# The first 60 microseconds of an attention and two-MLP kernel: tau waited for later, other pieces, another closing of the norms

## The reference, cut to what matters

```python
# q, k, v: [1, 6016, 256] fp32, tau a scalar
qn = q / (norm(q, axis=1) + 1e-6)          # one norm per channel, over the 6016 tokens
kn = k / (norm(k, axis=1) + 1e-6)
s  = kn.T @ qn / tau                        # 256 x 256 scores
a  = softmax(s, rows)
x  = v @ a                                  # [6016, 256]
g  = x @ w_gate; x = (silu(g) * (x @ w_val)) @ w_out       # 256 -> 1536 -> 256
h  = x @ w_in;   out = (h * clip(h + 3, 0, 6) / 6) @ w_out2 # 256 -> 2048 -> 256
```

## Time and profile before

| what | us |
|---|---|
| median of three runs | 1160.79 |
| the profiled execution's own time | 1160.25 |
| its span | 1158.5 |
| TensorE busy in the span | 1150.3 |
| DVE, ScalarE, GpSimd busy | 709.6, 270.6, 76.6 |

### The profile page before, as it was taken

The page is one execution under the profiler, slowest core; times in us unless marked ns, Lnnn a source line. Parts: engine busy times, 40 slices in busy tenths (PEclk is TensorE's granted clock), DMA queues, the critical chain, the costliest instruction groups (busy, mean ns, idle before and its releaser), DMA issues.

```text
span 1158.5 us, 14651 instructions
## 1 busy us (share of the span) xinstructions
PE 1150.3 (99%) x5222; PEld 965.3 (83%) x5222; DVE 709.6 (61%) x1167; ACT 270.6 (23%) x450; POOL 76.6 (7%) x48
## 2 busy tenths in 40 slices
PE   8999999999999999999999999999999999999999
PEld 7888888888888888888888888888888888888998
DVE  5776764664665574485485476466557447548557
ACT  6731211211221221221121121122122122112122
POOL 5794000000000000000000000000000000000000
PEclk9999999999999999999999999999999999999999
DMA  9742020010002002002002002000100200100100
GB/s 347 243 127 55 1 37 0 0 31 5 0 3 33 0 0 36 0 0 36 0 0 36 0 0 34 3 0 9 28 0 0 36 0 0 32 0 0 19 1 14
DMA packets 106048, 33.77 MB, mean 29 GB/s; under 512 B 95664, under 2 KB 100400, under 8 KB 106032
## 3 DMA queue, kind: packets, MB, share of 16 engines
q1 hardware_dynamic: 105024, 32.51, 11.2%
q10 hardware_dynamic: 1008, 1.05, 0.3%
HBM read 27.39 MB, written 6.16 MB: 29 GB/s over the span
## 4 chain that ended last, share of the span: by engine, by line
PE 96%; ACT 1%; DMA 1%; DVE 1%; issue 0%; SPq 0%; ACTq 0%
PE psum L751 33%; PE psum L774 32%; PE psum L762 22%; PE psum L786 5%; PE psum L734 1%; ACT psum L387 1%; PE psum L804 1%; DMA tau_sb<-in_tau 1%; PE psum L654 1%; DVE sq_sum L482 1%; PE psum L802 0%; DMA qk_first<-in_q 0%; PE psum L818 0%; ACT parts_early L383 0%; ACT parts_late L383 0%
## 5 line engine op out<-in xcount | busy, mean ns | idle before, releaser
L774 PE MATMUL psum<-prod,down_w 128*128 128x512 f32 (+1 forms) x1644 | 410.2, 387 | 0.0
L774 PEld LDWEIGHTS psum<-prod,down_w 128*128 128x128 f32 x1644 | 307.9, 188 | 61.8
L762 PE MATMUL psum<-yT,up_w 128*128 128x512 f32 (+1 forms) x1152 | 281.7, 385 | 0.0
L762 PEld LDWEIGHTS psum<-yT,up_w 128*128 128x128 f32 x1152 | 215.2, 188 | 41.8
L601 DVE TENSOR_TENSOR act_out<-psum,act_out 128x512 f32<-128x512 f32 (+1 forms) x144 | 97.9, 680 | 237.3 <-PE psum L751 237.1
L751 PE MATMUL psum<-vT,gate_w 128*128 128x512 f32 (+1 forms) x864 | 215.4, 384 | 0.0
L751 PE MATMUL psum<-vT,val_w 128*128 128x512 f32 (+1 forms) x864 | 215.4, 384 | 0.0
L441 ACT ACTIVATE act_out<-psum 128x512 f32<-128x512 f32 (+1 forms) x144 | 85.2, 591 | 470.5 <-PE psum L751 470.5
L751 PEld LDWEIGHTS psum<-vT,gate_w 128*128 128x128 f32 x864 | 161.3, 188 | 31.0
L751 PEld LDWEIGHTS psum<-vT,val_w 128*128 128x128 f32 x864 | 161.3, 188 | 30.9
L614 DVE SCALAR_TENSOR_TENSOR act_out<-act_out,psum 128x512 f32<-128x512 f32 (+1 forms) x192 | 129.0, 672 | 77.1 <-ACT act_out L449 77.0
(11 more groups left out here) (95 smaller groups left out, 376.7 us busy)
## 6 DMA issues: line engine op xcount, KB each, us to landing
out<-out_sb SPq DMA_DIRECT2D x45, 128.0 KB, 2.5
v_in<-in_v SPq DMA_DIRECT2D x44, 128.0 KB, 3.4
qk<-in_q SPq DMA_DIRECT2D x7, 512.0 KB, 9.0
qk<-in_k SPq DMA_DIRECT2D x7, 512.0 KB, 11.3
w_stage<-in_moe_w_out SPq DMA_DIRECT2D x7, 512.0 KB, 3.9
w_stage<-in_moe_w_in SPq DMA_DIRECT2D x4, 512.0 KB, 3.6
qk_more<-in_q SPq DMA_DIRECT2D x3, 512.0 KB, 11.2
qk_more<-in_k SPq DMA_DIRECT2D x3, 512.0 KB, 13.3
```

What stands on the lines that cost most here:

```text
L762: end = mm(HID[j % 4][:, 0:n], up2_w[:, part, b, j * P:(j + 1) * P], yT[:, m, b, 0:n], start=(part, m, b) == (0, 0, 0), stop=(part, m, b) ...
L774: end = mm(banks[h][:, 0:n], w[:, part, j, h * P:(h + 1) * P], prod[:, c % 4, m, 0:n], start=j == 0 and (part, m) == PASSES[0], stop=False)
```

## The change

1. The first piece is one DMA for q and one for k (256 KB each), segment 0 one each (512 KB), each waited for whole.
2. Segments 2 to 8 are split instead of 1 to 7. Segment 1 is multiplied wide, and segment 8's last two chunks go the split way.
3. DVE's wait for tau and `neg_tau` stand after the sums, ahead of the wait for the roots. The DMA itself is issued where it was.
4. Closing of the sums: the squares of segment 9's k go into a staging buffer for weights (`w_stage[:, 1]`), GpSimd folds their four chunks onto one, ScalarE copies that into PSUM, and DVE adds it last. DVE folds segment 9's q at once, then segment 10's q, the last chunk of both, and segment 10's k.
5. TensorE: segment 9 half 0 comes ahead of the last split part; q's norms stand between the two halves of segment 10 half 0, k's norms behind them; then segment 11 half 0, one product of segment 9 half 1, the scale products, and the rest as before. Seven products of the scores followed the scale products up to `turn_exp(0)`, now it is five.
6. The last cast of the up weights on ScalarE comes before the second exp.

```diff
-    SPLIT = range(1, 8)
+    SPLIT = range(2, 9)
@@ sync
-            for c in range(FIRST):
-                sp.dma_start(qk_first[:, 0, c * C:(c + 1) * C], q_seg[:, c * C:(c + 1) * C]).then_inc(first_loaded[c], 16)
-            load(sp, 0, 0, 0, WIDE * C, seg_loaded[0])
-            load(sp, 0, 0, WIDE * C, SEG * C, rest_loaded)
+            sp.dma_start(qk_first[:, 0, :], q_seg[:, 0:FIRST * C]).then_inc(first_loaded, 16)
+            load(sp, 0, 0)
...
             for n, (src, _, _) in enumerate(PIECES):
+                if n == 1:
+                    sp.wait_ge(k_folded_kept, 1)
@@ gpsimd, after the split parts
+            pool.wait_ge(squared, 2 * HALVED + 2)
+            for i, width in enumerate((2 * C, C)):
+                if i > 0:
+                    pool.wait_ge(k_folded, i)
+                nc.gpsimd.tensor_tensor(k_squares[:, 0:width], k_squares[:, 0:width], k_squares[:, width:2 * width],
+                                        ALU.add).then_inc(k_folded, 1)
@@ scalar
+                elif s == HALVED:
+                    nc.scalar.activation(k_squares, slot(s)[:, 1, :], ACT.Square).then_inc(squared, 1)
+                else:
+                    act.wait_ge(squares_added, SUMS)
+                    nc.scalar.activation(SQ_Q_END, slot(s)[:, 0, :], ACT.Square).then_inc(squared, 1)
+                    act.wait_ge(squares_added, Q_HALVED)
+                    nc.scalar.activation(SQ_K_END, slot(s)[:, 1, :], ACT.Square).then_inc(squared, 1)
...
-            for i in range(EARLY_CASTS):
+            cast_up(0)
+            act.wait_ge(k_folded, 2)
+            act.wait_ge(squares_added, Q_SUMMED)
+            nc.scalar.copy(K_PART, k_squares[:, 0:C]).then_inc(k_folded_kept, 1)
+            for i in range(1, EARLY_CASTS):
                 cast_up(i)
...
             expT_evict(0)
-            exponent(1)
             for i in range(EARLY_CASTS + MIDDLE_CASTS, len(UP_BLOCKS)):
                 cast_up(i)
+            exponent(1)
@@ vector
-            dve.wait_ge(tau_loaded, 16)
-            nc.vector.tensor_scalar_mul(neg_tau[:, :], tau_sb[:, :], -1.0)
...
+            added(sum_q[:, 0:half], SQ[0][:, 0:half], sum_q[:, 0:half])
+            added(SQ[0][:, half:], SQ[0][:, half:], sum_q[:, half:])
+            dve.wait_ge(squares_added, SUMS + 2)
+            added(sum_q[:, 0:half], SQ[0][:, half:], sum_q[:, 0:half])
+            dve.wait_ge(squared, 2 * FULL_SEGS - 1)
+            dve.wait_ge(squares_added, Q_HALVED)
+            added(sum_q[:, 0:half], SQ_Q_END[:, 0:half], sum_q[:, 0:half])
+            dve.wait_ge(squares_added, Q_HALVED + 1)
+            added(SQ_Q_END[:, half + C:], SQ_Q_END[:, half + C:], sum_q[:, C:half])
+            added(sum_q[:, 0:C], SQ_Q_END[:, half:half + C], sum_q[:, 0:C])
+            dve.wait_ge(squares_added, Q_HALVED + 3)
+            added(sum_q[:, 0:C], SQ_Q_END[:, half + C:], sum_q[:, 0:C])
...
+            added(sq_sum[:, :, 0:C], SQ_LAST, sq_sum[:, :, 0:C])
...
+            added(sum_k[:, 0:half], SQ_K_END[:, 0:half], sum_k[:, 0:half])
+            added(SQ_K_END[:, half:], SQ_K_END[:, half:], sum_k[:, half:])
...
+            added(SQ_K_END[:, half + C:], SQ_K_END[:, half + C:], sum_k[:, C:half])
+            added(sum_k[:, 0:C], SQ_K_END[:, half:half + C], sum_k[:, 0:C])
...
+            added(sum_k[:, 0:C], SQ_K_END[:, half + C:], sum_k[:, 0:C])
+            dve.wait_ge(k_folded_kept, 1)
+            dve.wait_ge(squares_added, K_SUMMED)
+            added(sum_k[:, 0:C], K_PART, sum_k[:, 0:C])
@@ tensor
+            wide(HALVED, range(SEG), (0,))
             split_part(SPLIT[-1])
-            wide(HALVED, range(SEG), (0,))
-            pe.wait_ge(squares_added, 2 * (FULL_SEGS - 1) + 8)
...
+            wide(HALVED + 1, range(WIDE), (0,))
+            pe.wait_ge(squares_added, LAST_ADDED)
+            norms_of(0)
+            wide(HALVED + 1, range(WIDE, SEG), (0,))
+            pe.wait_ge(squares_added, ALL_ADDED)
+            norms_of(1).then_inc(norms_summed, 1)
+            wide(SEGS - 1, range(LAST_CHUNKS), (0,), stop=True).then_inc(scores_summed, 1)
+            wide(HALVED, range(1), (1,))
...
             end.then_inc(scale_summed, 1)
-            wide(SEGS - 1, range(LAST_CHUNKS), (0,), stop=True).then_inc(scores_summed, 1)
-            wide(HALVED, range(SEG), (1,))
+            wide(HALVED, range(1, SEG), (1,))
             wide(HALVED + 1, range(WIDE), (1,))
```

More of the change, by code:

```diff
@@ L243, in attention_mlp_mlp_kernel, with load @@
         TURNED = (2, 4)
-        def load(queue, s, x, begin, end, loaded):
-            at = seg_at(s)
-            queue.dma_start(slot(s)[:, x, begin:end], (q_seg, k_seg)[x][:, at + begin:at + end]).then_inc(loaded, 16)
+        def load(queue, s, x):
+            at, width = seg_at(s), seg_chunks(s) * C
+            queue.dma_start(slot(s)[:, x, 0:width], (q_seg, k_seg)[x][:, at:at + width]).then_inc(seg_loaded[s], 16)
+        SUMS = 2 * HALVED
+        Q_HALVED, Q_SUMMED, LAST_ADDED, K_SUMMED, ALL_ADDED = SUMS + 3, SUMS + 7, SUMS + 8, SUMS + 13, SUMS + 14
+        SQ_Q_END, SQ_K_END, K_PART = SQ[1], SQ[0], SQ[1][:, 0:C]
+        k_squares = w_stage[:, 1, :]
         def slot(s):
@@ L358, in _ @@
         def _(act):
[L359 to L362, removed]
+            act.dma_start(qk_first[:, 1, :], k_seg[:, 0:FIRST * C]).then_inc(first_loaded, 16)
+            load(act, 0, 1)
             def table_of(function):
@@ L368, in _ @@
             table_of(ACT.Sqrt)
-            for c in range(FIRST):
-                act.wait_ge(first_loaded[c], 32)
+            act.wait_ge(first_loaded, 32)
             for h in range(2):
@@ L471, in _, with added @@
             nc.vector.memset(sq_sum[:, :, FIRST * C:SEG * C], 0.0).then_inc(sums_cleared, 1)
-            dve.wait_ge(tau_loaded, 16)
-            nc.vector.tensor_scalar_mul(neg_tau[:, :], tau_sb[:, :], -1.0)
             dve.wait_ge(first_squared, 2)
             dve.wait_ge(sums_cleared, 1)
-            for s in range(FULL_SEGS - 1):
+            def added(dst, a, b):
+                nc.vector.tensor_tensor(dst, a, b, ALU.add).then_inc(squares_added, 1)
+            for s in range(HALVED):
                 for h in range(2):
@@ L481, in _ @@
                         dve.wait_ge(squares_added, 2 * (s - 1) + h + 1)
-                    nc.vector.tensor_tensor(sq_sum[:, h, :], SQ[h], sq_sum[:, h, :], ALU.add).then_inc(squares_added, 1)
-            added = 2 * (FULL_SEGS - 1)
+                    added(sq_sum[:, h, :], SQ[h], sq_sum[:, h, :])
             half = 2 * C
-            for h in range(2):
-                dve.wait_ge(squared, 2 * (FULL_SEGS - 1) + h + 1)
-                dve.wait_ge(squares_added, 2 * (FULL_SEGS - 2) + h + 1)
-                nc.vector.tensor_tensor(sq_sum[:, h, 0:half], SQ[h][:, 0:half], sq_sum[:, h, 0:half],
-                                        ALU.add).then_inc(squares_added, 1)
-                nc.vector.tensor_tensor(SQ[h][:, half:], SQ[h][:, half:], sq_sum[:, h, half:],
-                                        ALU.add).then_inc(squares_added, 1)
@@ L502, in _ @@
[L502 to L508 removed]
+            sum_q, sum_k = sq_sum[:, 0, :], sq_sum[:, 1, :]
@@ L679, in _ @@
             stay_awake(AWAKE_START)
+            pe.wait_ge(first_loaded, 32)
             for c in range(FIRST):
-                pe.wait_ge(first_loaded[c], 32)
                 for h in range(KC):
                     product(h, qk_first[:, 0, c * C:(c + 1) * C], qk_first[:, 1, c * C:(c + 1) * C], start=c == 0)
-            wide(0, range(WIDE), range(KC))
-            pe.wait_ge(rest_loaded, 32)
-            wide(0, range(WIDE, SEG), range(KC)).then_inc(seg_multiplied, 1)
+            for s in range(SPLIT.start):
+                wide(s, range(SEG), range(KC)).then_inc(seg_multiplied, 1)
             for s in SPLIT:
```

56 lines of the change are left out of this document (25 added, 31 removed).

## The result

| | before | after |
|---|---|---|
| median of 17 runs each, us | 1160.24 (1158.59 to 1161.75) | 1157.68 (1157.36 to 1159.25) |
| the profiled execution's own time, its span | 1160.25, 1158.5 | 1157.67, 1155.9 |

The ratio is 0.9981 with a 95% interval of 0.9974 to 0.9989: 2.56 us between the medians. The forecast was 1159.5, its range 1158.2 to 1160.8.

The account below looks back on a forecast made before the run. TensorE, 99% busy, was taken as the bound, so only when it reaches the folds counted. `turn_exp(0)` 0.7 us earlier, 1.2 with 0.5 of earlier data, gave 1159.05, or 1159.6 off the median; it said 1159.5, range 1158.2 to 1160.8.

Parts of the forecast that it names:

- sign of being wrong: TensorE ahead of k's norms: the prediction is wrong if the gap there, 0.88 us before the change, remains.
- The split choice, 0.7 us on TensorE: Head on TensorE: segment 1 wide and segment 8 split puts it ahead by 0.65 to 0.75 us, taken as 0.7.
- Earlier data, "I take 0.5 us": First loads: whole pieces bring all later segments 0.5 us sooner, between bounds of nothing and 1.3 us.
- forecast without shift: The sum before any earlier data: segment 8's add ends at 35.05, all is added at 42.85.
- rival 1: Data come much earlier, or the casts don't hold up exp: up to 2.75 us gained, 1158.0; chance 0.18.
- Norms and TensorE move with it alike: Up to `turn_exp(0)`: 0.5 us of earlier data shifts norms and TensorE equally, so the gain is 1.2 instead of 0.7.
- DVE's closing isn't shortened by sharing it: Last adds of the sums on DVE: 7.8 us changed against 7.7 before, though three engines share the closing.
- Behind the norms: From norms to `turn_exp(0)`: 4.2 us, exp right behind the casts, TensorE standing some 0.7 to 0.8 us.
- GpSimd's cover: Split parts: GpSimd's low parts are ready 1 us before TensorE needs them, growing by 0.14 per segment.
- tau: priced too low: DVE's wait for tau, moved behind the adds: worth 0.1 to 0.4 us on DVE, nothing by itself on TensorE.
- Rival 4: DVE's adds: tau was the bound, so all moves by the 2 us DVE starts sooner, 1158.8; chance 0.05.
- Rival 3: TensorE waiting for whole segment 0: its clock falls to half, 3.1 us later, 1163.2; chance 0.05.

Follow-up runs that it names:

- Whole pieces alone: Kernel before with first piece and segment 0 each loaded as one DMA for q and one for k, all else as before: 1160.37 us, ratio 0.9997.
- segments 1 to 7 split: Changed kernel with segments 1 to 7 split instead of 2 to 8, segment 8 multiplied wide: 1157.52 us, ratio 0.9988 to the kernel before.
- tau late alone: Kernel before with only DVE's wait for tau and `neg_tau` moved behind the sums: 1158.68 us, ratio 0.9989.
- one cast less: Changed kernel with tau's DMA issued later and four up-weight casts before the root, one after, instead of three and two: 1156.28 us, ratio 0.9977 to the kernel before.
- the closing alone: Changed kernel with halved pieces, SPLIT range(1, 8) and tau waited for first, against the kernel before: 1158.12 us, ratio 0.9989.

## Why the prediction was right or wrong

**The point that sets the time.** In five profiles of the kernel before and the one of after, all with the clock held, the time less the start of `turn_exp(0)`'s matmuls is 1111.2 to 1111.3 us (1159.66 less 48.44, 1157.67 less 46.39). Behind this point nothing changes, as the prediction had it. Its sum of that point failed in one term, and the median it was set against held something that it never priced. Its own sign of being wrong, a gap before k's norms, is there: 0.55 us.

**Where the sum missed.** From the profile read to after, the norms end 1.65 us earlier (43.93 to 42.28), and `turn_exp(0)` follows them 0.82 us sooner (4.93 to 4.11): 2.47 in all. The forecast had 0.43 for the first (0.5 of data less 0.07) and 0.73 for the second, 1.2 in all. So the miss lies ahead of the norms.

**The split choice, 0.7 us on TensorE: right there, and worth nothing.** Whole pieces alone had segment 3 at 17.24, the changed kernel with data as early has it at 16.56: 0.68. But segments 1 to 7 split gave 1157.52 against 1157.68. The prediction carried the 0.7 to `turn_exp(0)` because the norms were to be ready first; they weren't.

**Earlier data, "I take 0.5 us": the step that failed.** Of the 2.74 us at segment 3, 2.05 are left for the data, and DVE's closing began 1.45 us earlier than the forecast without shift had it: the term was three to four times too small. In part that is the draw: segment 1 starts at 13.62 in the profile read, at 11.66 to 12.34 in four other profiles of the kernel before, at about 10.6 in after, and tau lands at 13.1 against 11.3 to 12.5. What whole pieces bring is some 1.2 at segment 1, near the upper bound of 1.3 that the prediction kept for rival 1. Less of it is left one segment on: with segments 1 to 7 split, segment 2 starts at 14.09 and 13.66 with whole pieces, and at 14.05 to 15.29 in six profiles with halved ones, the one read left out.

The reading behind the 0.5, that the low rate would stay as it did at 9 us, took two things for one. The low rate at 5 us goes with the halved first piece: 154 to 322 GB/s in the eight profiles that have it, 410 to 430 in the ten that don't. It is not the rate of its 1 KB rows, since none of them is under way at 5 us (of 126 packets in that microsecond of before, 113 are of 2 KB and more, and 13 under 512 B), and it begins before tau's DMA is issued at 4.4 (201 GB/s from 3.5 to 4 in tau late alone). How four small DMAs slow what comes behind them is open. The low rate at 9 us goes with tau's DMA, where the first piece is whole (111 to 168 GB/s in eight profiles, 414 and 422 in the two with that DMA late).

**"Norms and TensorE move with it alike": wrong, the data reach the norms only through DVE.** The closing began 1.45 us before the forecast without shift (33.60 against 35.05), not 2.05, and took 8.0 instead of 7.8. So k's norms had a wait of 0.55 where 0.65 was to spare. Of the 0.6 lost on the way, the trace shows ScalarE and with it DVE standing for a segment that lands late:

```profile
27.14 0.62 ACT L392 CAST parts_early<-qk 128x512 fp32r<-128x512 f32 x1 [0.58 <-DMA qk<-in_k]
```

In the ten profiles in which tau is waited for late, DVE waits so once between 24 and 29 us, for 0.51 to 1.76 us. In one stretch ahead of it there is a packet of another kind between the segments' (the queues of after from 22.9 to 24 us):

```profile
q1 hardware_dynamic: 119, 0.44, 98.9%
q8 instruction: 1, 0.02, 5.5%
```

That this fetch of instructions makes a segment land late is argued, not tested.

**DVE's closing isn't shortened by sharing it: right** (8.0 against 7.7). What the new order brings in time lies behind the norms: `turn_exp(0)` follows their end by 4.1 us in the profiles with it whose clock held (3.9 with one cast less), by 4.9 in those of the kernel before. In front of them TensorE has other work while DVE adds, and the clock holds more often. Between runs with the clock held the closing alone, with that order, gives 1158.12 against 1158.69 beside it.

**Behind the norms: right.** `turn_exp(0)` comes 4.1 us after their end (42.28 to 46.39; forecast 4.2), after a gap of 0.53 in the weight loads (0.7 to 0.8), with the exp right behind the casts. GpSimd's cover held: its last low parts end at 35.42, the split part that reads them starts at 37.14.

```profile
33.03 2.39 POOL L348 TENSOR_TENSOR parts_late<-qk,parts_late 128x1024 fp32r<-128x1024 f32 x1
```

**tau: priced too low.** The prediction set aside the chain through tau because DVE "has caught up with the data by the time that the closing begins". It had not: the 16 adds of the earlier trace rows run back to back, and in that profile neither DVE nor ScalarE waits for a segment behind 14 us. The first add waited for tau:

```profile
13.14 0.15 DVE L473 TENSOR_SCALAR neg_tau<-tau_sb 128x1 f32<-128x1 f32 x1 [11.04 <-DMA tau_sb<-in_tau]
```

In four of the five profiles of the kernel before the norms begin 29.74 or 29.75 us after this instruction (13.14, 12.51, 12.08 and 11.49), and so they do with whole pieces alone; in the fifth, where a segment landed late, 30.57 us. So tau's landing did bound the norms. Rival 4's 2 us aren't there all the same, since the next bound, the late segment above and ScalarE's pace, is near: in the kernel before waiting late is worth 0.5 us between runs with the clock held, in the changed one 0.2. It goes with fewer runs whose clock fell too, 1 of 11 against 15 of the 35 beside them, which chance could make. What tau costs besides is its DMA, 1.26 us in the changed kernel, which the prediction left at nothing because the change leaves it in place.

**The clock: the right cause at the wrong place.** Rival 3 had it fall at the wait for segment 0. There it was 1.00 in every profile, with waits of 1.16 us in after and up to 2.52 in others (weight loads). It falls behind the norms, in 37 of 105 runs of the kernel before (median 1160.94, against 1158.78 of the 68 others: 2.2 us; all runs of it beside the experiments, but for one whose clock record, 0.949, fits neither) and in 3 of 17 of the changed one (1158.65, 1158.82, 1159.25). The traces show 1.7 of the 2.2: with the old order the norms and what follows take 7.87 or 7.88 us up to `turn_exp(0)`'s matmuls where the clock fell, 6.19 or 6.20 where it held. With the new order k's norms and what follows take 5.68 against 4.72, 1.0 more. The Trainium skill, page "TensorE: Matmul & The Clock Gate", section "Part 1: The HAM clock gate (the "warmup" mystery)", has an idle array go to half its clock; the clock of 0.50 behind the waits agrees. The prediction's profile is one with the clock held and late data, 0.54 below the median shown; it took that median for more runs of the same kind, and so didn't see that part of it may be an event which the change can remove.

**The sum as it was.** With the clock held: 1158.78 before, 1157.67 after, 1.11 us. That this is near the 1.2 of the forecast is luck, for it is made up otherwise: some 0.6 from closing and order, the rest from data and tau together; the edits don't add. The other 1.45 of the 2.56 us are the kernel before's runs with late data or a fallen clock, which lift its median above 1158.78. The two can't be told apart in these 17 runs, whose clock is not on record. And early data without the new closing bring nothing at all (0.9997 and 1.0003): TensorE waits longer, and the clock falls more often.

## What to carry to other kernels

Before a forecast, put several executions of the kernel before side by side, and read the granted clock of each: a median may hold an event (here a fall of the clock, 1.7 us in a third of the runs) that one profile doesn't show, and one profile may have late data that the next one doesn't. Where an engine's work runs back to back behind one wait, that wait sets its end, whatever the rates say of its having caught up. A gain upstream of a wait goes into that wait, and if the engine is TensorE it can cost its clock as well; so give it real work to do there first, and then bring the data sooner. A transfer of a few bytes per partition belongs where the large ones beside it are not waited for at once, not where its issue happens to be free: here it went beside the loads of weights and v.

## What the hardware showed that was not expected

- TensorE ran at half its clock for some 3 us behind waits of 1.25, 1.50, 1.61 and 2.81 us before the one-column products, and at full clock behind waits of 1.04, 1.30 and 1.82 us: no bound on the wait separates them. Filling 2.4 us of such a wait took the fallen runs from 10 of 11 to 0 of 11.
- In eight profiles with a whole first piece, 128 four-byte elements under way go with a rate of 111 to 168 GB/s from 9 to 10 us, and in the two with that DMA late it is 414 and 422; against 418 GB/s the three microseconds of after lack some 1.3 us of transfer (an estimate from 299, 135 and 254). With a halved first piece the same elements passed beside 400 to 422 GB/s in five of eight profiles.
- Behind a first piece in four DMAs with rows of 1 KB the rate falls at 3.5 us and stays low until 7, though those rows are through by 4 (231 against 422 GB/s at 5 us), while the halved pieces of segment 0, rows of 2 KB, do not delay segment 1 (10.53).
